# Where the second half's outputs are summed, when the first block's activations are split, and when the second unit's weights are loaded

## The reference, cut to what matters

```python
x = attention(q, k, v, s)            # 4 batches x 8 heads, 576 positions, head size 64, causal, with a bias from s
x = x.transpose(0, 2, 1, 3).reshape(2304, 512)
h = maximum(maximum(x @ w1, x @ w2), x @ w3)    # 512 -> 768
y = h @ w_out                                   # 768 -> 512
return (y @ w_a) * (y @ w_b) @ w_out2           # 512 -> 1536 -> 512
```

## Time and profile before

| | us |
|---|---|
| median of 3 timed runs | 982.69 (979.66, 982.69, 982.72) |
| the profiled execution | 980.57 |
| its span, first to last instruction | 978.8 |
| PE busy | 920.4 (94%) |
| DVE busy | 676.1 (69%) |
| ACT busy | 482.4 (49%) |
| POOL busy | 349.6 (36%) |

### The profile page before, as it was taken

One profiled execution on the slowest core, in us unless ns is written; L12 is line 12 of the kernel. 1 busy time (PEld: TensorE's weight loads), 2 busy tenths in 40 slices (PEclk: granted clock), 3 DMA queues, 4 the chain that ended last, 5 costly groups with the idle time before them and its releaser, 6 DMA issues.

```text
span 978.8 us, 16853 instructions
## 1 busy us (share of the span) xinstructions
PE 920.4 (94%) x5992; PEld 903.2 (92%) x5992; DVE 676.1 (69%) x1369; ACT 482.4 (49%) x1071; POOL 349.6 (36%) x453
## 2 busy tenths in 40 slices
PE   3789899999999999999979899998999998999998
PEld 2588889999999999999979899998999998999998
DVE  6789788877666677563353598994688883688850
ACT  4778677676655556543232354442344442344420
POOL 6868654444433423411010443440144340234300
PEclk9999999999999999999999999999999998999999
DMA  3644322222221221100020333221221211121101
GB/s 114 225 152 138 96 86 71 69 74 78 64 80 39 84 65 46 53 4 27 12 108 14 130 132 97 72 70 49 93 79 61 65 44 57 52 60 50 43 1 65
DMA packets 32225, 71.42 MB, mean 73 GB/s; under 512 B 3600, under 2 KB 18032, under 8 KB 32112
## 3 DMA queue, kind: packets, MB, share of 16 engines
q1 hardware_dynamic: 32144, 70.36, 22.7%
HBM read 60.40 MB, written 9.88 MB: 72 GB/s over the span
## 4 chain that ended last, share of the span: by engine, by line
PE 85%; DVE 7%; issue 3%; ACT 2%; DMA 1%; POOL 1%; SPq 0%; DVEq 0%; ACTq 0%; POOLq 0%
PE bank L1409 24%; PE bank L1284 23%; PE bank L1416 14%; PE bank L1304 8%; PE bank L1235 6%; PE bank L1265 6%; PE bank L1251 5%; DVE w_lo_even L983 1%; DVE g_lo L1172 1%; ACT yt_hi L784 1%; DVE yt_lo L1002 0%; DMA y_raw<-in_w 0%; POOL soft L547 0%; DVE soft L937 0%; DMA qk_st<-cum_row 0%
## 5 line engine op out<-in xcount | busy, mean ns | idle before, releaser
L1284 PE MATMUL bank<-xs_hi,w_hi 128*128 128x256 f32 (+1 forms) x576 | 174.7, 303 | 7.3 <-ACT m_tmp L647 5.2
L547 POOL TENSOR_SCALAR soft<-soft,rden 128x576 f32<-128x576 f32 (+4 forms) x160 | 102.2, 658 | 216.1 <-DVE rden L923 216.1
L1284 PE MATMUL bank<-xs_hi,w_lo 128*128 128x256 f32 (+1 forms) x576 | 171.4, 297 | 0.0
L1284 PE MATMUL bank<-xs_lo,w_hi 128*128 128x256 f32 (+1 forms) x576 | 171.2, 297 | 0.0
L1284 PEld LDWEIGHTS bank<-xs_hi,w_hi 128*128 128x128 f32 x576 | 109.9, 191 | 9.0 <-issue 6.2
L937 DVE CUSTOM_DVE_ANT_0 soft<-bank,causal 64x576 f32<-64x576 f32 (+4 forms) x160 | 85.3, 540 | 46.4 <-PE bank L1235 45.1
L618 ACT ACTIVATE soft<-soft,neg_max 64x576 f32<-64x576 f32 (+4 forms) x160 | 96.0, 600 | 35.7 <-DVE neg_max L937 34.5
L1284 PEld LDWEIGHTS bank<-xs_lo,w_hi 128*128 128x128 f32 x576 | 110.2, 191 | 1.1
L1284 PEld LDWEIGHTS bank<-xs_hi,w_lo 128*128 128x128 f32 x576 | 110.0, 191 | 0.0
L946 DVE TENSOR_TENSOR pt_lo<-bank,pt_hi 128x320 fp32r<-128x320 f32 (+4 forms) x160 | 76.1, 489 | 47.4 <-ACT pt_hi L625 45.5
L1235 PE MATMUL bank<-qk_st 128*128 128x256 f32 (+4 forms) x384 | 93.1, 359 | 16.1 <-DMA qk_st<-cum_row 13.7
(11 more groups left out here) (127 smaller groups left out, 2237.9 us busy)
## 6 DMA issues: line engine op xcount, KB each, us to landing
qk_raw<-in_qk SPq DMA_DIRECT2D x32, 576.0 KB, 3.9
raw_even<-in_w SPq DMA_DIRECT2D x18, 512.0 KB, 3.8
raw_odd<-in_w SPq DMA_DIRECT2D x17, 512.0 KB, 3.5
w_raw<-in_w SPq DMA_DIRECT2D x16, 384.0 KB, 3.8
v_raw<-in_v SPq DMA_DIRECT2D x32, 160.0 KB, 2.2
y_raw<-y_dram SPq DMA_DIRECT2D x3, 1536.0 KB, 7.3
outT<-o_stage SPq DMA_DIRECT2D x24, 192.0 KB, 1.9
qk_raw<-in_qk SPq DMA_DIRECT2D x8, 256.0 KB, 3.2
```

The source lines that it names most:

```text
L547: nc.gpsimd.tensor_scalar(part, part, rden[n % 2][:, i:i + 1], 1.0, ALU.mult, ALU.mult).then_inc(prob_done, 1)
L1284: ins = nc.tensor.matmul(up_ps[g][:, 0:width1(c)], up1_w(w, f, g, kc), x[:, kc, 0:width1(c)], start=(kc == 0 and at == 0), stop=(kc == KC ...
```

## The change

1. The right half's outputs 1 to 3 sum in the product banks 1 to 3 instead of banks 4 to 6. PE no longer waits for `o_ready` before them, but for `c22_done`, `c21_done` and `c12_done` of the last unit, and in the next block's first unit P2, P4 and P3 each wait until the output in their bank has been copied out.
2. The splits of block 0's activations are spread: sums and the first three of seven in slot 46, the other four in slot 47, each behind the slot's first `m_copy` and `h_lo_sub`. Unit 0's weights are split in slot 48.
3. SP issues the loads of the weights of units 1 and 2 in slot 48 before the last four stores.
4. In the first unit of a block ACT runs `q_copy` before the weight copies. In all units ACT runs `u_copy` before weight part 2, and DVE runs `c21` and `c22` before weight part 2 and before the down weights.

```diff
-        late_ps = [sum_ps] + out_ps[0:KC - 1]
+        late_ps = [sum_ps, r0_ps, r1_ps, r2_ps]
...
+                if early == 3:
+                    load_w2(1)
+                    load_w2(2)
                 c, e = place(n)
                 if STEPS - 1 in downs_of(n):
                     for j in range(KC):
                         store_y(c, j)
 
-            load_w2(1)
             load_wd(1)
-            load_w2(2)
...
-                if early == 1:
-                    y_hi_copies(0)
                 exp(n, 0)
...
+                    if i == 1 and early in (1, 2):
+                        y_hi_copies(0, Y_ORDER[0:3] if early == 1 else Y_ORDER[3:])
+                    if i == 0 and early == 3:
+                        for part in range(3):
+                            w2_hi_copy(0, part)
...
+                if t == 0:
+                    q_copy(u)
                 if u + 1 < N_CH2 * UNITS:
                     w2_hi_copy(u + 1, 0)
                     w2_hi_copy(u + 1, 1)
-                q_copy(u)
+                if t > 0:
+                    q_copy(u)
+                if odd:
+                    g_hi_copy(u, 0)
+                u_copy(u)
                 if u + 1 < N_CH2 * UNITS:
                     w2_hi_copy(u + 1, 2)
...
-                if early == 1:
-                    y_sums(0)
-                    y_lo_subs(0, Y_ORDER)
                 neg_scores(n, 1)
...
+                    if early == 1 and i == 0:
+                        y_sums(0)
+                    if early in (1, 2) and i == 2:
+                        y_lo_subs(0, Y_ORDER[0:3] if early == 1 else Y_ORDER[3:])
...
-                    for part in range(3):
-                        w2_lo_sub(u + 1, part)
+                    w2_lo_sub(u + 1, 0)
+                    w2_lo_sub(u + 1, 1)
                 if odd:
                     g_lo_sub(u, 0)
+                c21(u)
+                c22(u)
+                if u + 1 < N_CH2 * UNITS:
+                    w2_lo_sub(u + 1, 2)
+                if odd:
+                    g_lo_sub(u, 1)
                 if u < FB2:
                     wd_lo_sub(u)
-                c21(u)
-                c22(u)
-                if odd:
-                    g_lo_sub(u, 1)
...
                 need(pe, c22_done, u)
+                if t == 0:
+                    need(pe, o_ready[1], 2 * c)
                 product(u, P2, r0_ps, True)
...
                 for j in range(1, KC):
-                    pe.wait_ge(o_ready[j - 1], 2 * c + 1)
+                    pe.wait_ge((c22_done, c21_done, c12_done)[j - 1], u + 1)
                     second_half(c, j, range(FB2))
```

More of the change, by code:

```diff
@@ L758, in slot @@
                             x_hi(ahead, kc)
+                    if i == 1 and early in (1, 2):
[3 more added lines that the diff above has]
+                            w2_hi_copy(0, part)
                 if downs:
                     y_copy(c, KC - 1)
-                if early == 2:
-                    for part in range(3):
-                        w2_hi_copy(0, part)
             def w2_hi_copy(u, part):
@@ L772, in w2_hi_copy, with y_hi_copies @@
                                      ).then_inc(w2_hi_done, 1)
-            def y_hi_copies(c):
+            def y_hi_copies(c, xs):
                 act.wait_ge(y_loaded, 16 * (c + 1))
@@ L778, in y_hi_copies @@
                 sums = {P6: 2, P4: 4, P7: 3, P5: 1}
-                for x in Y_ORDER:
+                for x in xs:
                     if x in sums:
@@ L846, in unit @@
                 if odd:
-                    g_hi_copy(u, 0)
+                    g_hi_copy(u, 1)
                 if u < FB2:
                     wd_hi_copy(u)
-                u_copy(u)
-                if odd:
-                    g_hi_copy(u, 1)
             def out_copy(c, half, j):
@@ L877, in _ @@
                 if c + 1 < N_CH2:
-                    y_hi_copies(c + 1)
+                    y_hi_copies(c + 1, Y_ORDER)
                 for half in range(2):
@@ L1105, in slot @@
                             x_lo(ahead, kc)
+                    if early == 1 and i == 0:
+                        y_sums(0)
+                    if early in (1, 2) and i == 2:
+                        y_lo_subs(0, Y_ORDER[0:3] if early == 1 else Y_ORDER[3:])
+                    if early == 3 and i == 0:
+                        for part in range(3):
+                            w2_lo_sub(0, part)
                 if len(rows) == 2:
@@ L1111, in slot @@
                     max_2(c, rows[-1])
-                if early == 2:
-                    for part in range(3):
-                        w2_lo_sub(0, part)
             for n in range(N_SLOTS):
@@ L1459, in unit @@
                 need(pe, c21_done, u)
+                if t == 0:
+                    need(pe, o_ready[2], 2 * c)
                 product(u, P4, r1_ps, True)
@@ L1467, in unit @@
                 need(pe, c12_done, u)
+                if t == 0:
+                    need(pe, o_ready[3], 2 * c)
                 product(u, P3, r2_ps, True)
```

## The result

| | before | after |
|---|---|---|
| median of the timed runs | 981.20 (979.66 to 982.72, 4 runs) | 955.02 (954.78 to 955.06, 4 runs) |
| the profiled execution, its span | 980.57, 978.8 | 955.04, 953.3 |

The account below looks back on a forecast made before the run. PE bounds the kernel (85% of the last chain), so its stops count: four gaps 24.5 us, plus 1.8 for u_sb, minus 1.0 at P7, gives 25.3 off 980.57; forecast 955.5 us, 8-in-10 range 952 to 963.5.

Parts of the forecast that it names:

- A: PE's stop in slot 46, waiting for ACT's m_tmp: 6.9 us lost, forecast to go whole.
- D: PE's stop at the end of block 1, waiting for ACT's o_stage: 6.5 us lost, forecast to go whole.
- C: PE's stop at the end of block 0, waiting for ACT's o_stage: 5.5 us lost, forecast to go whole.
- B: PE's stop in unit 0 of block 0, waiting for ACT's q_sb: 5.6 us lost, forecast to go whole.
- Edit 2: Spread splits in slots 46 to 48: A goes at no cost, max_1 about 1.4 us early in slot 47.
- Edit 3: Early weight loads and q_copy first: unit 1's weights ready 4 us ahead of unit 0, so B goes.
- B goes twice over: Unit 0 of block 0: early load and q_copy(0) passing the weight copies both counted as removing the 5.6 us stop.
- Edit 4, the cost: P7 of block 0's five even units starts later, 0.2 us each, 1.0 in all; nothing in blocks 1 and 2.
- Edit 4, the gain: P2 of units 2, 14 and 26 waits for u_sb 1.9 us in all; 1.8 taken as gained.
- The rival of the port: DVE becomes the bound in even units, its operations lengthened by POOL at a shared port: 960.5 to 963.5 us, chance 0.15.
- The signs named beforehand: After slot 45: listed gap waits gone, clock 1.00, P7 waits of 0.1 to 0.3 us, no u_sb wait over 0.2.
- The slow pace: 8.1 us of slow matmuls behind the four gaps goes with them; rival that it stays: 963.4 us, chance 0.05.

Follow-up runs that it names:

- e2: Kernel before, banks still shared, with ACT's two copies of the left half's outputs moved ahead of its seven activation copies: 971.06 us.
- e3: Changed kernel with all seven splits of block 0's activations in slot 46, DVE's low parts ahead of the second row's maximum: 957.73 us.
- e5: Changed kernel with the loads of units 1 and 2 back behind the last stores, q_copy first kept: 959.58 us.
- e6: Changed kernel with q_copy back behind the two weight copies in unit 0, early load kept: 955.42 us.
- e9: Changed kernel with q_copy ahead of the two weight copies in every even unit: 954.14 us.
- e11: Changed kernel with one more 512-column DVE operation in every odd unit, ahead of weight part 2: 960.92 us.
- r1: The changed kernel itself run again, nothing altered: 955.36 us.
- e8: Changed kernel with the order within a unit undone on ACT and DVE, except q_copy first in unit 0: 958.65 us.
- the second group: Runs on one chip: the changed kernel again (955.36 us), e5, e6 and e9, with the kernel before beside them (982.45 us).
- e10: Kernel before with POOL's sums cut to 16 of 256 columns from unit 4 on: 975.16 us.
- e1: Kernel before with only the right half's outputs 1 to 3 moved to the product banks: 969.93 us.
- e4: Changed kernel with block 0's activation splits all back in slot 46 ahead of the first m_copy and maximum: 961.88 us.
- e7: Changed kernel with the loads back behind the last stores and q_copy back behind the weight copies: 960.81 us.

## Why the prediction was right, point by point

- **Gaps A to D.** Forecast 6.9, 5.6 and 12.0 for C with D; undone or done alone they measured 6.5, 5.45 and 12.7. Pricing a gap from the last matmul before it to the first at full pace again was right: the waits alone would have given 5.2, 3.7 and 7.5. That the prices agree to 0.7 is in part luck, since the length of the slow pace changes from execution to execution: in the profiles that still have the gap, A lost 6.7 to 8.1 us behind the same wait of 5.2, and B 5.3 to 6.9 behind 3.6 to 4.1.
- **C and D, the cause.** The place in ACT's queue, as said; e2 shows that the shared banks were not needed for the loss.
- **Edit 2.** There is no wait, with 1.6 us to spare before the maximum (e3), where 1.4 was forecast.
- **Edit 3.** The sum was right, the reason too generous. "B goes twice over" is wrong: the load takes all of it, `q_copy(0)` first takes 1.2 of 5.45 by itself and 0.06 beside the load (e5, e6). Without the early load the stop only moves on to units 1 and 2, in three pieces.
- **Edit 4, the cost.** Forecast: five times 0.2 at P7 in block 0, nothing in blocks 1 and 2. The trace has five times 0.23, and e9 takes them away by moving `q_copy` alone. The spare of 0.5 in the other blocks is borne out (e11). The sixth stop of 0.31 us in r1 is not in the sum.
- **Edit 4, the gain.** This term was mis-sized, in two ways. I took the waits for `u_sb` from the list, 1.9, and did not price them by the starts as I did the gaps; by the starts the same three stops cost 0.44, 1.04 and 1.20 us in the kernel before, 2.7 together. And with the other edits in, they are larger: e8 has four stops of 4.6 us together, and the medians say about the same (3.3 net, plus the 1.15 paid). The order of before then meets POOL's sums otherwise: the listed waits are 1.5 and 1.6 us in units 14 and 26 in place of 0.8 and 0.9.
- **Why the total came out all the same.** In one profiled execution against the other, the gain is 980.57 - 955.04 = 25.5, where 25.3 was forecast. The traces split it. Gap A gave 6.9. From the first matmul of the last layer to the last one, PE took 434.3 us before and 415.4 after: 18.9, where the forecast had 5.6 + 12.0 + 1.8 - 1.0 = 18.4. The stretch before gap A, which the change leaves alone, took 0.35 longer in the execution after. So the forecast had the gain at `u_sb` 0.9 too small and the price at P7 0.15 too small, and the longer first stretch, which is chance, took back 0.35: the closeness of the total is partly luck. The parts undone one at a time sum to 12.7 + 6.5 + 5.45 + 3.3 = 28, and the medians of the second group differ by 27.1.
- **The rival of the port.** The forecast that POOL does not meet the moved operations was right in its direction and too timid. They don't meet: weight part 2 takes 952 and 947 ns in the mean after the change and the down weights 682, as with POOL's narrow sums in e10 (958 and 685). Besides, some operations that met before no longer do: with the order of before (e8) DVE is busy 35 us more. (A few meet newly, and it costs PE nothing: the low parts of the activations take 1091 ns in the mean where they took 952.) That POOL is the cause is shown by e10. My length of an operation that meets nothing, 631 ns, is 684 in e10: 384, 512 and 768 columns take 552, 684 and 958 there, so a share of 768 columns leaves out a fixed part, by these numbers about 0.14 us. The Trainium skill, SBUF — State Buffer, section "SBUF: two separate sides", has the loser of the shared port pair block fully. The traces bear out that an operation of DVE gets longer beside a sum of POOL, with 1164 against 684 ns; whether it stands still for a time or runs slowly throughout, they don't tell. The rule spoke against the change in the prediction, and turned out to speak for it.
- **The signs named beforehand.** POOL's first sum for unit 1 starts before unit 0, no wait for `u_sb` is in the list, and the 168 matmuls behind the last product of block 0 run without a stop. The stops before P7 have the forecast size, but the list of waits, where I wanted to see them, doesn't have them.
- **The slow pace** went with the gaps, as forecast. My reason, that the low clock shows only behind gaps of over 3.7 us, does not hold: e10 has it behind 2.34 us once and not behind 2.35.

## What to carry to other kernels

Price a stop of PE by the starts of its matmuls, from the last before it to the first at full pace, and not by the list of waits, which left out a third of the loss at the four gaps and did not show the stops of 0.12 us at all. Where two engines lengthen each other's operations, ask of each reordering which operations it takes out of the other engine's time as well as which it puts there; the same three operations took 3.24 or 3.78 us, with POOL's last sum 1.2 us later beside the second. And where a result waits in the queue of a copying engine behind copies for later use, moving just that copy ahead is the cheapest cure: two copies were worth 11.5 us in e2, and one per even unit the last 1.2 in e9.

## What the runs showed of the hardware that I had not expected

- DVE's and POOL's busy times are not a sum of their work. One order of the same instructions gave DVE 337.45 us in the last stretch, another 301.99. In these traces it strikes operations that read no PSUM bank. In the kernel before, between 545 and 950 us, the 50 additions of 384 columns that read a bank while a sum of POOL ran took 0.54 to 0.56 us, as they did without one; of the 46 `g_lo` of the same size that ran beside a sum, and read no bank, 24 took 1.09 or more, and without a sum all took 0.54 to 0.56.
- The kernel before spreads over 979.66 to 983.45 us in its timed runs, the changed one over 954.78 to 955.53, e10 (narrow sums, the four gaps still there) over 974.47 to 975.69. Part of it goes with the gaps: the slow pace behind gap A ended 3.5 us after the restart in the profiled execution of before, 6.0 after it in those of e1 and e2 (6.9 against 8.1 us lost), with the same wait of 5.2. e4 and e7 point the same way: each has the DVE times of the changed kernel and one gap left, and one of its four runs lies 1.7 or more above the others. Whether POOL's sums meet DVE otherwise from run to run was not followed.
- In e1 the record of the granted clock lies at 0.95 from about 60 us on, and the pace of the matmuls is the usual one (its last layer, less its stops, takes 414.1 us; that of the kernel after 414.2), with as many in a stretch as the kernel before has there (116 in 20 us):

```profile
600.00:620.00 20.00, 20.00 (x116) 0.95 0.29 88
```

So a clock of 0.95 in the record says nothing of the pace by itself; the starts do. (At 970.75 us this is the slowest of e1's four executions, with one of the longer slow stretches behind A.) Why it reads so in this one execution stays open.
- Also open is what decides whether a stop of 2.1 to 2.4 us is followed by the slow pace, and how long that lasts: of three such stops (e3, and two in e10), one was.
